# Twelve output units in one run a step: the second layer of a two-scale attention and MoE kernel

## The reference, cut to what matters

```python
def _moe2_ref(x, w_in, w_out):      # x 2304 x 512, w_in 512 x 2048, w_out 2048 x 512
    h = x @ w_in
    g = h * np.cos(h)
    return (g @ w_out).astype(np.float32)
```

## Time and profile before

| | |
|---|---|
| median of three runs | 685.02 us (684.56 to 686.89) |
| the profiled execution's own time | 684.41 us |
| its span | 682.6 us |
| second layer in it | from 292.8 us to the end |
| TensorE busy | 672.1 us, 98% |
| VectorE busy | 435.7 us, 64% |
| ScalarE busy | 404.5 us, 59% |
| GpSimd busy | 205.8 us, 30% |

### The profile page before, as it was taken

The page is one execution under the profiler, slowest core; times in us unless marked ns, Lnnn a source line. Parts: engine busy times, 40 slices in busy tenths (PEclk is TensorE's granted clock), DMA queues, the critical chain, the costliest instruction groups (busy, mean ns, idle before and its releaser), DMA issues.

```text
span 682.6 us, 12769 instructions
## 1 busy us (share of the span) xinstructions
PE 672.1 (98%) x4767; PEld 597.6 (88%) x4767; DVE 435.7 (64%) x828; ACT 404.5 (59%) x849; POOL 205.8 (30%) x301
## 2 busy tenths in 40 slices
PE   7899999999999999999999999999999999999998
PEld 4677889889889898999999988999889998899986
DVE  7888965665662233358787879966655676555563
ACT  5678865565664655566566656654544766444544
POOL 6988754554523555402122231400000000000000
PEclk9999999999999999999999999999999999999999
DMA  8962422222000000546434445443322336332202
GB/s 303 321 203 83 150 81 76 78 76 76 26 1 1 1 1 1 184 140 238 164 139 180 177 149 206 137 171 109 109 108 108 120 127 244 141 111 108 108 2 92
DMA packets 18446, 82.78 MB, mean 121 GB/s; under 512 B 1872, under 2 KB 5968, under 8 KB 15056
## 3 DMA queue, kind: packets, MB, share of 16 engines
q1 hardware_dynamic: 18384, 81.96, 34.2%
HBM read 62.56 MB, written 19.40 MB: 120 GB/s over the span
## 4 chain that ended last, share of the span: by engine, by line
PE 93%; DVE 2%; POOL 2%; issue 1%; ACT 1%; POOLq 0%; ACTq 0%; DVEq 0%
PE ps L1640 29%; PE ps L1617 26%; PE ps L1505 15%; PE ps L1474 13%; PE ps L1489 2%; PE ps L1446 1%; PE ps L1396 1%; PE ps L1381 1%; PE ps L1432 1%; PE ps L1421 1%; PE ps L1406 1%; PE ps L1514 1%; DVE soft L1097 0%; DVE pr L1101 0%; DVE w_split L1158 0%
## 5 line engine op out<-in xcount | busy, mean ns | idle before, releaser
L1617 PE MATMUL ps<-y_parts,w_parts 128*128 128x384 f32 x1008 | 184.8, 336 | 0.0
L1617 PEld LDWEIGHTS ps<-y_parts,w_parts 128*128 128x128 f32 x1008 | 177.3, 188 | 3.8 <-ACT part L946 0.2
L1640 PE MATMUL ps<-wo,g_hi 128*128 128x512 f32 x576 | 178.2, 390 | 0.0
L1640 PEld LDWEIGHTS ps<-wo,g_hi 128*128 128x128 f32 x576 | 107.5, 188 | 20.6
L1640 PE MATMUL ps<-wo,g_lo 128*128 128x512 f32 x288 | 113.0, 392 | 0.0
L1284 DVE TENSOR_TENSOR h<-ps,part 128x384 f32<-128x384 f32 x72 | 40.1, 556 | 99.6 <-PE ps L1617 99.3
L1505 PE MATMUL ps<-ln_hi,w_split 128*128 128x384 f32 x384 | 103.3, 339 | 0.0
L946 ACT ACTIVATE part<-ps 128x384 f32<-128x384 f32 x72 | 35.2, 489 | 70.7 <-PE ps L1617 70.6
L1474 PE MATMUL ps<-w_split,x_hi 128*128 128x512 f32 x288 | 72.8, 395 | 0.7 <-DVE xT L1152 0.5
L1505 PEld LDWEIGHTS ps<-ln_hi,w_split 128*128 128x128 f32 x384 | 69.8, 188 | 0.0
L977 ACT ACTIVATE g_hi<-turn 128x384 fp32r<-128x384 f32 x96 | 49.8, 519 | 24.5 <-DVE turn L1298 24.5
(11 more groups left out here) (114 smaller groups left out, 950.4 us busy)
## 6 DMA issues: line engine op xcount, KB each, us to landing
w_parts<-w_kept SPq DMA_DIRECT2D x16, 1792.0 KB, 7.4
w_kept<-w_parts SPq DMA_DIRECT2D x8, 1792.0 KB, 6.7
qk_in<-in_qk SPq DMA_DIRECT2D x16, 586.0 KB, 4.4
vblk<-in_v_blocks SPq DMA_DIRECT2D x16, 384.0 KB, 5.7
v<-in_v_rows SPq DMA_DIRECT2D x16, 288.0 KB
result<-o_sb SPq DMA_DIRECT2D x18, 256.0 KB, 5.9
xT<-in_w_in SPq DMA_DIRECT2D x8, 512.0 KB, 8.0
raw_wo<-in_w_out SPq DMA_DIRECT2D x8, 512.0 KB, 9.0
```

Source lines behind the costliest of these rows:

```text
L1617: last = nc.tensor.matmul(product_ps(s, k), w[:, m, a, c, :], y_parts[:, n, b, c, :], start=(not adds and c == 0 and m == 0 and n == 0), s ...
L1640: last = nc.tensor.matmul(o_ps(tile), g[n][:, t * P:(t + 1) * P], wo[:, p, w, f, :], start=(first and m == 0), stop=(done and m == 2))
```

## The change

The twelve units of a step are put behind P3 in one run, so that P4 of the step before and P1, P2, P6, P5, P7, P3 follow each other. ScalarE's and VectorE's orders of a step are rewritten. Nothing else changes: the same instructions, buffers, semaphores and waits.

```diff
-UNITS = (0, 0, 6, 0, 0, 6, 0)
+UNITS = (0, 0, 0, 0, 0, 12, 0)
```

VectorE's:

```diff
-                if s:
-                    times_cos(s - 1, 1)
                 add_corner(s, 0)
                 if s:
                     fraction(s - 1, 3)
                     split_g(s - 1, 1)
                     times_cos(s - 1, 2)
-                fraction(s, 0)
+                add_corner(s, 1)
                 if s:
                     times_cos(s - 1, 3)
+                fraction(s, 0)
+                if turns:
+                    split_y(q + 1, B11)
+                if s:
+                    split_g(s - 1, 2)
                 if s + 1 < JOINS:
                     split_w(s + 1, False)
                 if s:
-                    split_g(s - 1, 2)
-                add_corner(s, 1)
+                    split_g(s - 1, 3)
                 if turns:
-                    split_y(q + 1, B11)
-                if s:
-                    split_g(s - 1, 3)
+                    split_y(q + 1, B21)
+                fraction(s, 1)
+                if s + 1 < JOINS:
+                    split_w(s + 1, True)
+                add_corner(s, 2)
                 if 2 <= s <= 5:
                     split_wo(s + 2)
-                add_corner(s, 2)
+                if turns:
+                    split_y(q + 1, T2)
                 times_cos(s, 0)
-                fraction(s, 1)
-                if turns:
-                    split_y(q + 1, B21)
                 if q and j == 0:
                     split_y(q, T4)
+                fraction(s, 2)
+                times_cos(s, 1)
                 if turns:
-                    for piece in (T2, T1, T3):
-                        split_y(q + 1, piece)
+                    split_y(q + 1, T1)
+                    split_y(q + 1, T3)
                 split_g(s, 0)
-                fraction(s, 2)
                 if turns:
                     split_y(q + 1, B22)
-                if s + 1 < JOINS:
-                    split_w(s + 1, True)
             s = STEPS - 1
-            times_cos(s, 1)
             fraction(s, 3)
```

More of the change, by code:

```diff
@@ L1011, in _ @@
                     to_turns(s - 1, 3)
+                    cosine(s - 1, 2)
+                    split_g(s - 1, 1)
+                copy_part(s, P6)
+                if s == 0:
+                    copy_x2(GROUPS - 1, 1)
+                copy_part(s, P5)
+                if s:
+                    cosine(s - 1, 3)
                 if opens:
                     copy_out(q - 1, 2)
-                    copy_out(q - 1, 3)
-                if s:
-                    split_g(s - 1, 1)
+                to_turns(s, 0)
+                if s == 0:
+                    copy_x2(GROUPS - 1, 2)
+                else:
+                    split_g(s - 1, 2)
                 if s + 1 < JOINS:
@@ L1020, in _ @@
                     split_y(q + 1, B11)
+                if s:
+                    split_g(s - 1, 3)
+                if turns:
+                    split_y(q + 1, B21)
                 if 2 <= s <= 5:
                     split_wo(s + 2)
-                if s:
-                    cosine(s - 1, 2)
-                if turns:
-                    split_y(q + 1, B21)
+                if opens:
+                    copy_out(q - 1, 3)
+                to_turns(s, 1)
                 if opens:
                     copy_out(q - 1, 4)
[L1030 to L1036, removed]
-                    split_g(s - 1, 2)
-                copy_part(s, P5)
+                if s + 1 < JOINS:
+                    split_w(s + 1, True)
                 if turns:
                     split_y(q + 1, T2)
-                if s:
-                    split_g(s - 1, 3)
-                if s + 1 < JOINS:
-                    split_w(s + 1, True)
-                cosine(s, 0)
+                if opens:
+                    copy_out(q - 1, 5)
                 if q and j == 0:
                     split_y(q, T4)
-                if opens:
-                    copy_out(q - 1, 5)
+                cosine(s, 0)
                 if turns:
                     split_y(q + 1, T1)
[L1054 to L1059, removed]
                 to_turns(s, 2)
+                cosine(s, 1)
                 if q and j == 0:
@@ L1063, in _ @@
                 if turns:
+                    split_y(q + 1, T3)
                     split_y(q + 1, B22)
-                cosine(s, 1)
+                split_g(s, 0)
                 if q and j == 0:
@@ L1070, in _ @@
             to_turns(s, 3)
+            cosine(s, 2)
             split_g(s, 1)
-            cosine(s, 2)
             cosine(s, 3)
```

1 line of the change is left out of this document (removed).

## The result

The changed kernel takes 687.38 us (median of 8 runs, 686.57 to 687.97), the kernel before 685.03 (8 runs): a ratio of 1.0034, 95% interval 1.0025 to 1.0043. It is slower by 2.35 us, just over the 0.3% that the prediction took as what a measurement can tell; forecast was +1.4. Two executions in the experiments lie far out, 1346.2 us in experiment 8 and 3794.8 us in experiment 9, and are left out there.

A forecast was written before the change was run, and what follows sets the result against it. TensorE, busy 98% of the span at full clock, was taken to bound the kernel. Terms -1.3 - 0.2 (P3's old wait) + 2.5 + 0.2 + 0.2 gave +1.4: 686.4 us against the median, range 683.3 to 688.8.

The forecast's parts named there:

- Switches, -1.3: On TensorE, one pair of product and unit runs fewer in 23 steps, 0.055 us each: -1.3 us (0 to -1.8).
- Rival E: Switches between products and units are free, so nothing is saved there: +2.7, 687.7 us, slower; chance 0.08.
- The run of seven and the room of 0.05 behind P2's add: Seven products end to end; P5, now directly behind P2's add, keeps 0.05 us before its weight load: cost nothing.
- Rival D: P2's add is late in every step, 0.1 us in 23 steps on top: +3.7, 688.7 us; chance 0.07.
- ScalarE's order at nothing: ScalarE's rewritten order in a step delays no copy of a product, with 0.36 us of room before P6: cost 0.
- Step 6 to 7, +2.5: GpSimd's y differences hold four VectorE operations ahead of P2's add, so P5 and P7 wait: +2.5 us (0 to +3).
- Rival B: No step crossing is exposed to GpSimd's work, nothing is late: -1.5, 683.5 us; chance 0.20.
- list of signs that it is wrong altogether: In the profile after: a gap before a unit or at P1 or P4, or a clock below the top level.
- Step 8 to 9, +0.2: GpSimd's second group of y differences catches three VectorE operations, not four, as whole(2) is let through: +0.2 us (0 to +2).
- rival C: Step 8 to 9 catches four VectorE operations as well, one more at 2.0 us: +3.4, 688.4 us, slower; chance 0.13.
- Step 0 to 1, +0.2: GpSimd's w sums catch one or two VectorE operations before g_lo(0), making P6's copy late: +0.2 us (0 to +0.8).
- case A: The forecast itself: one step crossing exposed to GpSimd's work, +1.4 us, within 0.3%; chance 0.52.

The follow-up runs named there:

- experiment 8: The version of experiment 6 with three units put behind P6 and nine behind P3, instead of twelve in one run: 685.75 us, ratio 1.0012 to the kernel before.
- experiment 9: The version of experiment 6 with 2, 4, 6 and 8 needless VectorE operations ahead of P2's add in steps 10, 13, 16 and 19: 693.48 us.
- experiment 6: Changed kernel, pass 1 y differences on VectorE, pass 2's one a step, step 0's w halves split before P7's add: 683.09 us, 0.9973 to the kernel before.
- experiment 7: The kernel before with twelve units in one run but its old ScalarE and VectorE orders, save three copies of results: 709.52 us, ratio 1.0354.
- experiment 2: Changed kernel with GpSimd's four pass 2 y differences each waiting for VectorE's end of step, one a step: 686.87 us, ratio 1.0032 to the kernel before.
- experiment 5: Changed kernel with three of the twelve units put behind P6 as cover, nine left behind P3: 688.39 us, ratio 1.0049 to the kernel before.

## Why the prediction was right, and where it was off

**Switches, -1.3.** Right: 15.57 to 15.51, -1.5; experiment 8 shows it by itself. Rival E is out.

**The run of seven and the room of 0.05 behind P2's add.** Right, which by so thin a margin was partly luck: in plain steps nothing waits, in the changed kernel and in experiment 6; PEld waits for VectorE's h once in the layer, not twenty times. Rival D is out.

**ScalarE's order at nothing.** Right, and experiment 7 shows what it is worth.

**Step 6 to 7, +2.5.** The mechanism was right by its row: four operations held, the add 2.1 late and the copy of P6 behind it, 2.4 in all. Rival B is out. Missing was what such a wait does to TensorE itself. Every slice of the trace before had the clock at the upper level, and "the later one counts" ended the sum with the length of the wait. A clock below the top level was on the prediction's own list of signs that it is wrong altogether; it came. The effect of waits on the clock was put at nothing without a reason, and by the profiled execution that is 1.35.

**Step 8 to 9, +0.2.** Right: 0.3. `whole` of corner 2 was let through, with GpSimd starting at 435.44, and three were held; rival C is out.

```profile
435.28 0.35 DVE L1285 TENSOR_SCALAR whole<-turn 128x384 f32<-128x384 f32 x1
435.66 2.08 DVE L1288 TENSOR_TENSOR turn<-turn,whole 128x384 f32<-128x384 f32 x1
437.67 2.20 DVE L1294 TENSOR_TENSOR turn<-h,turn 128x384 f32<-128x384 f32 x1
439.79 2.19 DVE L1304 TENSOR_TENSOR g_lo<-turn,g_hi 128x384 fp32r<-128x384 f32 x1
```

**Step 0 to 1, +0.2.** 0.4: the right place and chain (g_lo(0), turns(3), P6's copy, P7), mis-sized. Behind step 0 VectorE had three operations lengthened by GpSimd's sums by some 1.3 in all (0.68, 0.98 and 1.09 where 0.35, 0.56 and 0.55 are usual), not one or two.

**The numbers.** +2.35 against +1.4, with 687.38 within 683.3 to 688.8. The case held most likely, A, is the one that came by its mechanism. But it was forecast to lie within 0.3% (0.66 for all such cases), and it came out just above, where the prediction gave 0.29, mostly to C, D and E. The missing clock term makes the difference: the two runs with a mean clock of 1.0 average 686.76, 1.7 over the kernel before. That the time lay within the range even so is no merit of case A, as the upper end of the range was set for the rivals; the time alone would fit E (687.7) better, and only the steps of 15.51 tell them apart.

## What to carry to other kernels

Where an order takes away cover, look for what moves at the same time as the covered operation: GpSimd's work held VectorE for 8 us in the kernel before too, and it cost 0.2 as long as units stood ahead of the product that waits. Cover placed ahead of a product also delays whatever that product starts; it helps only against delays that do not hang on it. And in a kernel that is all TensorE, mend the last waits of about two microseconds, and shorter ones that stand close together, before the others, as some of them cost the clock as well.

## What was not expected of the hardware

A wait of TensorE of about 2.1 to 2.3 us brought its clock to the lower level in some cases and not in others: in the profiles of the changed kernel and of experiment 2, not in that of experiment 5, and behind one of six equal waits in one execution. By the mean clock, which does not tell the place, it was 6 of 8 runs of the changed kernel, 4 of 6 of experiment 2 and none of 6 of experiment 5. What decides between them is open. The profiles only show that in the second layer it did not fall after a wait of 1.9 us or less that stood alone, and that a low stretch there cost about 1.35 to 1.6 us, except in experiment 7, where it lasted 7 us and cost some 2.8 (6 product matmuls in 2.29 and the 36 unit matmuls in 10.05, for 1.31 and 8.20).

A subtraction of GpSimd takes 1.84 us where VectorE is idle (experiments 2 and 6) and about 2.0 beside a held operation of VectorE (8.01 for four, 5.90 for three), while VectorE's 0.35 to 0.55 become 1.96 to 2.20: in this pairing VectorE pays almost all.
